# Experts' first layer: the last 64 features as two 64-row matmuls on the two halves of the array, with a double buffer for the transposed tile

## The reference, cut to what matters

```python
for b in range(B):
    for s in range(S):
        ...
        h = np.maximum(x[b, s] @ w1[e], 0.0)
        out[b, s] = p[e] * (h @ w2[e])
```

## Time and profile before

| | |
|---|---|
| runs of the kernel before | 1017.14 us median of 3 (1016.87 to 1017.91) |
| the profiled execution | 1017.4 us; its span 1015.7 us |
| TensorE busy | 974.8 us (96%) |
| VectorE, ScalarE, GpSimd busy | 482.5, 262.9, 270.7 us |
| mean granted TensorE clock | 0.983 |
| the experts' stage | from 693.99 us to the end, 31 tiles |

### The profile page before, as it was taken

One profiled execution on the slowest core, in us unless ns is written; L12 is line 12 of the kernel. 1 busy time (PEld: TensorE's weight loads), 2 busy tenths in 40 slices (PEclk: granted clock), 3 DMA queues, 4 the chain that ended last, 5 costly groups with the idle time before them and its releaser, 6 DMA issues.

```text
span 1015.7 us, 51867 instructions
## 1 busy us (share of the span) xinstructions
PE 974.8 (96%) x23581; PEld 773.1 (76%) x23582; DVE 482.5 (48%) x998; ACT 262.9 (26%) x441; POOL 270.7 (27%) x297
## 2 busy tenths in 40 slices
PE   4789999999999999999999999999999999999996
PEld 3679999999998995555555555558889888888884
DVE  6447887788778853223133133162452332323230
ACT  1134444444444442202202202202111111111110
POOL 4435556655665540000020020020151010110101
PEclk9589999999999999999999999999999999999999
DMA  5225433333333321940110110139131111001000
GB/s 143 63 76 183 143 109 108 100 99 110 111 115 94 102 65 45 313 138 1 39 40 1 39 40 0 50 110 319 41 105 33 34 33 32 22 27 39 21 27 3
DMA packets 56903, 80.58 MB, mean 79 GB/s; under 512 B 22114, under 2 KB 36910, under 8 KB 56848
## 3 DMA queue, kind: packets, MB, share of 16 engines
q1 hardware_dynamic: 32816, 58.08, 18.4%
q10 hardware_dynamic: 21008, 13.06, 5.0%
q0 software_dynamic: 3024, 8.72, 2.4%
HBM read 66.99 MB, written 14.45 MB: 80 GB/s over the span
## 4 chain that ended last, share of the span: by engine, by line
PE 94%; issue 2%; DVE 1%; DMA 1%; ACTq 0%; POOL 0%; ACT 0%; POOLq 0%; DVEq 0%
PE ps_D L1442 13%; PE ps_D L199 12%; PE ps_G L1431 8%; PE ps_E L1431 8%; PE ps_B L209 5%; PE ps_E L928 5%; PE ps_G L180 3%; PE ps_E L180 3%; PE ps_G L188 3%; PE ps_E L188 3%; PE ps_D L1011 3%; PE ps_A L902 3%; PE ps_E L926 3%; PE ps_D L962 3%; PE ps_B L902 2%; PE ps_D L902 2%
## 5 line engine op out<-in xcount | busy, mean ns | idle before, releaser
L1442 PE MATMUL ps_D<-room,hT 128*128 x496 | 138.7, 433 | 0.8 <-issue 0.8
L199 PE MATMUL ps_D<-room 128*128 128x384 f32 x384 | 126.3, 488 | 0.7 <-DVE room L264 0.7
L1442 PEld LDWEIGHTS ps_D<-room,hT 128*128 128x128 f32 x496 | 91.8, 190 | 35.7 <-issue 1.3
L199 PEld LDWEIGHTS ps_D<-room 128*128 128x128 f32 x384 | 72.4, 190 | 50.4 <-DVE room L264 1.3
L1393 POOL DMA_INDIRECT out<-y,token x31 | 30.7, 990 | 279.0 <-DVE y L1549 244.7
L522 POOL DMA_INDIRECT sorted_rows<-rows,slot x24 | 24.1, 1004 | 286.3 <-DVE slot L514 280.2
L866 POOL TENSOR_TENSOR room<-room 32x256 f32<-32x256 f32 x96 | 69.4, 723 | 106.3 <-DVE room L1282 100.9
L1532 DVE COPY w_own<-room 128x1024 f32 x62 | 43.5, 701 | 104.7 <-PE ps_G L1431 58.9
L1431 PEld LDWEIGHTS ps_G<-xTt,w_own 128*128 128x128 f32 x744 | 87.7, 192 | 5.3 <-ACT xTt L1478 0.9
L1431 PE MATMUL ps_G<-xTt,w_own 128*128 128x128 f32 x744 | 88.3, 275 | 0.6 <-ACT xTt L1478 0.6
L1431 PE MATMUL ps_E<-xTt,w_own 128*128 128x128 f32 x744 | 88.1, 275 | 0.0
(11 more groups left out here) (211 smaller groups left out, 1526.5 us busy)
## 6 DMA issues: line engine op xcount, KB each, us to landing
room<-in_moe_w SPq DMA_DIRECT2D x8, 1280.0 KB, 12.9
room<-in_moe_w SPq DMA_DIRECT2D x8, 1024.0 KB, 9.5
room<-in_kb SPq DMA_DIRECT2D x48, 160.0 KB
room<-in_vt SPq DMA_DIRECT2D x24, 320.0 KB, 3.0
x_in<-sorted_rows ACTq DMA_DIRECT2D x27, 161.0 KB, 2.2
room<-in_w SPq DMA_DIRECT2D x48, 82.7 KB
room<-in_a SPq DMA_DIRECT2D x48, 80.0 KB
room<-in_r SPq DMA_DIRECT2D x48, 80.0 KB
```

The source lines that it names most:

```text
L199: mm = pe.matmul(self.vs_bank[n % 2][:, 0:TH], self.v[:, s, d * P:(d + 1) * P], self.wspT[:, s, t * TH:(t + 1) * TH], start=(s == 0), stop ...
L1442: mm = pe.matmul(self.ps_y, side.hT[:, u % 2, f, :], self.weights.w2[:, bass.ds(e, 1), f, :], start=(f == 0), stop=(f == self.NF - 1))
```

## The change

`hidden` runs only two of the three matmuls of each block with 128 rows. The third becomes a matmul of 64 rows that lies on one half of the array's rows: partitions 0 to 63 for the blocks of bank G, 64 to 127 for those of bank E. They come behind all full matmuls, alternating between the halves. Their weights are copied to `w1_rest_own` as they lie, in one copy of 128 x 512, and the transposed features are put on both halves of the partitions, by two copies of 64 x 128. `xTt` has two buffers, and `turn_x(1)` moves ahead of `hidden(0)`. `relu` starts when the whole of `hidden` is done.

```diff
-        self.w1_own, self.hT = sb("w1_own", NK, E_FF), sb("hT", 2, E_FF // P, P)
+        self.w1_own, self.hT = sb("w1_own", NK - 1, E_FF), sb("hT", 2, E_FF // P, P)
+        self.w1_rest_own = sb("w1_rest_own", E_FF // 2)
...
-        self.xTt, self.y = sb("xTt", NK, P), sb("y", 2, DM)
+        self.xTt, self.y = sb("xTt", 2, NK, P), sb("y", 2, DM)
...
     def hidden(self, pe, turn, u):
 
         side, t = self.side, turn * self.SLOTS + u
+        x = side.xTt[:, u % 2]
         pe.wait_ge(self.xt_out, self.FREE + t + 1)
         for half in range(2):
-            pe.wait_ge(self.w1_in, 2 * t + half + 1)
+            pe.wait_ge(self.w1_in, 3 * t + half + 1)
             pe.wait_ge(self.h_out, self.FREE + 2 * t + half - 1)
             for f in range(4):
                 col = (half * 4 + f) * P
-                for k in range(NK):
-                    mm = pe.matmul(self.ps_h[half][:, f, :], side.w1_own[:, k, col:col + P], side.xTt[:, k, :],
-                                   start=(k == 0), stop=(k == NK - 1))
+                for k in range(NK - 1):
+                    mm = pe.matmul(self.ps_h[half][:, f, :], side.w1_own[:, k, col:col + P], x[:, k, :],
+                                   start=(f == 0 and k == 0), stop=False, skip_group_check=True)
             mm.then_inc(self.h_made, 1)
+        pe.wait_ge(self.w1_in, 3 * t + 3)
+        for f in range(4):
+            for half in range(2):
+                kept = slice(half * self.REST, (half + 1) * self.REST)
+                mm = pe.matmul(self.ps_h[half][:, f, :], side.w1_rest_own[kept, f * P:(f + 1) * P], x[kept, NK - 1, :],
+                               start=False, stop=True, skip_group_check=True)
+        mm.then_inc(self.h_made, 1)
...
-            if i == 3:
-                self.turn_x(pe, 0, 0)
+            if i >= 3 and i < 5:
+                self.turn_x(pe, 0, i - 3)
...
-        pe.wait_ge(self.padded, 1)
         self.hidden(pe, 0, 0)
         routing.turn_rows(pe, self.LAST)
-        self.turn_x(pe, 0, 1)
...
     def turned_x(self, act, turn, u):
-        t = turn * self.SLOTS + u
+        t, x, full, rest = turn * self.SLOTS + u, self.side.xTt[:, u % 2], NK - 1, slice(P - self.REST, P)
         act.wait_ge(self.xt_made, t + 1)
-        act.activation(self.side.xTt[:, :, :], self.ps_x, ACT.Copy).then_inc(self.xt_out, 1)
+        act.activation(x[:, 0:full, :], self.ps_x[:, 0:full, :], ACT.Copy)
+        act.activation(x[0:self.REST, full, :], self.ps_x[rest, full, :], ACT.Copy)
+        act.activation(x[rest, full, :], self.ps_x[rest, full, :], ACT.Copy).then_inc(self.xt_out, 1)
 
     def relu(self, act, turn, u):
         t = turn * self.SLOTS + u
         act.wait_ge(self.y_out, self.FREE + t - 1)
+        act.wait_ge(self.h_made, 3 * t + 3)
         for half in range(2):
-            act.wait_ge(self.h_made, 2 * t + half + 1)
...
         for half in range(2):
             cols = slice(half * 512, (half + 1) * 512)
-            if not isinstance(turn, int) or t >= 1:
-                dve.wait_ge(self.h_made, 2 * t + half - 1)
-            dve.tensor_copy(side.w1_own[:, 0:NK - 1, cols],
-                            w1.w1[:, bass.ds(e, 1), :, cols].rearrange("p o k f -> p (o k) f"))
-            kept = slice(half * self.REST, (half + 1) * self.REST)
-            dve.tensor_copy(side.w1_own[P - self.REST:, NK - 1, cols],
-                            w1.w1_rest[kept, bass.ds(e, 1), :].rearrange("p o f -> p (o f)")
-                            ).then_inc(self.w1_in, 1)
+            if later:
+                dve.wait_ge(self.h_made, 3 * t + half - 2)
+            dve.tensor_copy(side.w1_own[:, :, cols],
+                            w1.w1[:, bass.ds(e, 1), :, cols].rearrange("p o k f -> p (o k) f")).then_inc(self.w1_in, 1)
+        if later:
+            dve.wait_ge(self.h_made, 3 * t)
+        dve.tensor_copy(side.w1_rest_own[:, :], w1.w1_rest[:, bass.ds(e, 1), :].rearrange("p o f -> p (o f)")
+                        ).then_inc(self.w1_in, 1)
...
-        dve.memset(self.side.w1_own[0:P - self.REST, NK - 1, :], 0.0).then_inc(self.padded, 1)
```

More of the change, by code:

```diff
@@ L673, in all_stages @@
         fwd, bwd, starts = sb("fwd", WCOLS), sb("bwd", WCOLS + 1), sb("chunk_starts", WCOLS)
-        sb = Carver(side.w1_own.rearrange("p k f -> p (k f)"), 0, NK * E_FF)
+        sb = Carver(side.w1_own.rearrange("p k f -> p (k f)"), 0, (NK - 1) * E_FF)
         woutT, wgl = sb("woutT", NK, D_HALF), sb("wgl", NK, EXPERTS + 1)
@@ L1345, in __init__ @@
         self.h_made, self.h_out = sem("eh_made"), sem("eh_out")
-        self.w1_in, self.padded = sem("w1_in"), sem("padded")
+        self.w1_in = sem("w1_in")
         self.y_made, self.y_out = sem("y_made"), sem("y_out")
@@ L1503, in scalar @@
             gated.copy_out(act, self.LAST, i)
-            if i == 3:
-                self.turned_x(act, 0, 0)
+            if i >= 3 and i < 5:
+                self.turned_x(act, 0, i - 3)
         self.relu(act, 0, 0)
-        self.turned_x(act, 0, 1)
         routing.copy_rows(act, self.LAST)
@@ L1527, in fetch_w1 @@
         w1.until_loaded(dve, e)
+        later = not isinstance(turn, int) or t >= 1
         for half in range(2):
             cols = slice(half * 512, (half + 1) * 512)
-            if not isinstance(turn, int) or t >= 1:
-                dve.wait_ge(self.h_made, 2 * t + half - 1)
-            dve.tensor_copy(side.w1_own[:, 0:NK - 1, cols],
-                            w1.w1[:, bass.ds(e, 1), :, cols].rearrange("p o k f -> p (o k) f"))
-            kept = slice(half * self.REST, (half + 1) * self.REST)
-            dve.tensor_copy(side.w1_own[P - self.REST:, NK - 1, cols],
-                            w1.w1_rest[kept, bass.ds(e, 1), :].rearrange("p o f -> p (o f)")
-                            ).then_inc(self.w1_in, 1)
+            if later:
[6 more added lines that the diff above has]
+                        ).then_inc(self.w1_in, 1)
     def tile_dve(self, dve, turn, u):
```

## The result

| | kernel before | changed kernel |
|---|---|---|
| median of the runs side by side | 1017.0 us (1016.18 to 1017.91, 4 runs) | 1000.24 us (999.01 to 1001.21, 4 runs) |
| the profiled execution | 1017.4 us, span 1015.7 | 1001.21 us, span 999.5 |
| `hidden(2)` starts | 710.68 us | 709.87 us |
| a tile in the loop | 9.99 us | 9.45 to 9.50 us |

The account below looks back on a forecast made before the run. TensorE's own work was taken as the bound (busy 974.8 of 1015.7 us). A lead of 1.08 us at `hidden(2)` plus 29 tiles at 0.535 (15.5) gives 16.6 us: 1017.1 - 16.6 = 1000.5 us, range 993 to 1005.

Parts of the forecast that it names:

- Pairs at once: 64-row part of `hidden`: both row halves run together, 8 slots of 0.1125 us instead of 16, saving 0.88 us a tile.
- 5% longer than the ideal: L1011's 64-row matmuls: a slot of four takes 58.4 ns against 55.7, read as four array quarters working at once.
- The first rival: 64-row part: pairs don't overlap or loads don't hide, 16 records stay at 1.78 us; 1026.9 us, chance 0.07.
- The price of the change of mode: TensorE switching between 128 and 64 rows: 0.095 + 0.10 us going in, 0.095 + 0.055 coming out, 0.345 a tile.
- The tile: One tile on TensorE: 0.88 - 0.345 = 0.535 us less, from 9.99 to about 9.45 us.
- The other engines are covered: ScalarE's last copy done at about +2.9 us, due at +4.64, 1.7 to spare; VectorE covered too; cost nothing.
- The lead at `hidden(2)`: First tiles: `hidden(2)` starts at about 709.6 instead of 710.68 us, 1.08 us earlier.
- with two buffers and `turn_x(1)` moved ahead of `hidden(0)` this wait goes: Before the second `hidden`: TensorE's 0.63 us wait for the copy to `xTt` disappears.
- the 0.9 us: Before `hidden(2)`: TensorE waits 0.9 us idle for VectorE's copy of weights.

Follow-up runs that it names:

- Experiment 7: Changed kernel with the two 64 x 128 copies to `xTt` cut into 64 copies of 4 columns a tile; 1049.16 us, one run.
- experiment 1: Changed kernel with the same eight 64-row matmuls ordered as four of bank G, then four of E; 1016.86 us, ratio 1.0002.
- experiment 2: Changed kernel with the 64-row matmuls in the order G, G, E, E, twice; 1004.19 us, ratio 0.9869.
- experiment 3: Changed kernel with the 64-row part cut in two pieces, so twice as many changes of mode a tile; 1012.23 us, ratio 0.9951.
- experiment 5: Changed kernel with the two 64 x 128 copies to `xTt` cut into 8 copies a tile; 1002.91 us, one run.
- experiment 6: Changed kernel with the two 64 x 128 copies to `xTt` cut into 16 copies a tile; 1002.49 us, one run.
- experiment 8: Changed kernel with two sets of PSUM banks for `hidden`, two for `project`, and tile 2's weights copied before the routing's scan; 1000.28 us, ratio 0.9825.
- experiment 9: Kernel of experiment 8, with tile 6's weights also copied before the routing's last steps on VectorE; 998.69 us, ratio 0.9809.
- experiment 4: Changed kernel with the second tile's transposes back behind `hidden(0)`, double buffer kept; 1001.64 us, one run.

## Why the prediction was right

**Pairs at once: right.** Eight slots from the first pair to the last, 0.11 us each; the forecast was 0.1125. The evidence for it was weaker than the prediction took it to be, and that the slot came out so near is partly luck. The prediction counts L1011 as 64 columns, but only its weights have 64; 32 columns run through (the 64x32 in the earlier trace rows). A record with 128 columns takes 0.1115 us and one of `project` with 320 takes 4.31 / 16 = 0.269; on the line through these two, one with 32 would take about 0.03 us alone (an estimate), not 0.056. Records 0.0146 us apart then show some two at once, not four, so they leave open whether the row halves overlap, and "5% longer than the ideal" has no ground. The changed kernel's own rows show that they do. The first rival (load and matmul of a half in turn) is refuted by the 0.11 us between records on the same half.

**The price of the change of mode: right, and confirmed by doubling it.** Forecast 0.345 us a tile; the tile shows 0.10 + 0.10 on the way in and 0.10 + 0.05 on the way out. The 0.15 us that were too much around L902 were the only sign of it in the trace of before.

**The tile: 0.535 forecast, 0.53 measured** as the mean of 28 tiles (0.54 in the tile shown, 9.99 to 9.45). That makes 15.4 of the 15.5 us.

**The other engines are covered: right in the loop.** Forecast for the end of the last copy +2.9 us, measured +2.30; `relu` of bank G starts only 0.11 us behind the transposes, not 0.2, and a small copy follows the other without the gap that I had allowed. Experiment 7 shows that the limit lies where the prediction put it (+4.64 forecast, +4.46 measured).

**The lead at `hidden(2)`: 1.08 forecast, 0.81 measured, and by another way.** `hidden(0)` started at 694.67 and not at 694.32; this comes from ahead of the changed place, where the start of `hidden(0)` scatters from 693.65 to 695.30 us among the kernels of experiments 1 to 3, 5, 6, 8 and 9, which are alike up to there but for ScalarE's small copies and the banks. The step that failed is "with two buffers and `turn_x(1)` moved ahead of `hidden(0)` this wait goes". The wait for `xTt` went, but `hidden(1)` also needs bank G, which `relu` of tile 0 empties. That `relu` now starts at 699.61, behind the whole of `hidden(0)`, and ends at 700.21; `hidden(1)` starts at 700.35. I had followed the delay of `relu` to ScalarE's later work and to `project`, but not to the next writer of its bank. In the loop `project` lies between and hides it; between `hidden(0)` and `hidden(1)` there is no `project`. The sum hardly suffered, since the 0.9 us were booked in front of `hidden(2)`: having waited at `hidden(1)`, TensorE arrives there when VectorE's copy of 709.02 has just delivered the first half. Experiment 8 takes the bank's wait away, and it is gone.

What remains open: in the traces of experiments 1 to 6 and 8 the scaling of tile 3's result starts 1.5 to 2.1 us late, each time with a remote releaser; in those of the changed kernel and of experiments 7 and 9 it doesn't. About 7 us of routing steps stand behind it on VectorE, ahead of the weights of tile 6. In experiments 2, 4, 5 and 8 `hidden(6)` starts 0.81 to 1.06 us late, in experiments 3 and 6 0.23 and 0.28, in experiment 1 not at all. Experiment 7 is the same edit as 5 and 6 and doesn't have the late signal, so it hardly comes from one of the edits, but that isn't shown. What makes it late wasn't tested, nor whether it comes in every execution of a kernel.

## What to carry to other kernels

Matmuls that use half of the rows can be run in pairs, and a pair costs as much as one; but the two halves must lie close together in the program (in turn is best; two and two cost 0.10 us more, four and four lost the whole gain), and they should come in one piece, since each way in and out of the mode costs 0.15 to 0.20 us. One way in and out, 0.345 us, is the price of three slots of 0.11 us: here four pairs of fp32 matmuls a piece (eight slots) brought 0.54 us, two pairs a piece (experiment 3) only 0.15 in the whole tile. And when the reader of a buffer is delayed, ask who writes that buffer next at every place of the program, the first tiles too, not only in the steady loop.

## What the runs showed of the hardware

- TensorE starts a matmul on free rows ahead of up to three records that stand before it in the program and go to the other half; what stands farther back doesn't start (experiments 1 and 2). This is what two orders showed, with 64-row fp32 matmuls of 128 columns, each half writing a PSUM bank of its own. Whether the matmul or its weight load sets this reach, and whether two halves overlap into one bank, no run shows.
- The weights of a half are loaded while the same half multiplies: 0.11 us from record to record with a load of 0.19 us each (the weight loads of L1440 in the changed kernel). Only the first after a change of mode, or after a break in the alternation, isn't hidden; it is seen as a record of 0.37 instead of 0.27 us.
- A ScalarE copy from PSUM of 64 partitions and 4 to 32 columns right behind another costs 0.06 us (experiments 5 to 7), although its record is 0.18 to 0.25 us long.
